# Splitting the first feed-forward network's weights on GpSimd: half a chunk in each attention step of the first batch

## What is computed

```
attn_out = sm_attn(means of 4 rows of q, k, v), each row repeated 4 times
         + local attention over |i - j| < 4                # 4 batches x 8 heads x 576 x 64
x = attn_out as 2304 x 512
h = x @ w_in;  g = max(h, 0) + alpha * min(h, 0);  x = g @ w_out      # 512 -> 2048 -> 512
h = x @ w2_in; g = where(h > 0, h, exp(min(h, 0)) - 1); out = g @ w2_out
```

## Time and profile before

| | us |
|---|---|
| median of 3 runs | 921.67 |
| lowest and highest | 920.73, 924.37 |
| the profiled execution | 921.41 |
| its span | 919.6 |
| PE busy in the span | 906.8 |
| DVE, ACT, POOL busy | 541.3, 339.1, 281.3 |

### The profile page before, as it was taken

One profiled execution on the slowest core, in us unless ns is written; L12 is line 12 of the kernel. 1 busy time (PEld: TensorE's weight loads), 2 busy tenths in 40 slices (PEclk: granted clock), 3 DMA queues, 4 the chain that ended last, 5 costly groups with the idle time before them and its releaser, 6 DMA issues.

```text
span 919.6 us, 15263 instructions
## 1 busy us (share of the span) xinstructions
PE 906.8 (99%) x5611; PEld 850.2 (92%) x5616; DVE 541.3 (59%) x1071; ACT 339.1 (37%) x784; POOL 281.3 (31%) x399
## 2 busy tenths in 40 slices
PE   8799999999999999999999999999999999999998
PEld 6689999999999999999999998888888888988887
DVE  6665656555655554454455575656865657756563
ACT  6763335334534232241232142323442324423233
POOL 3799882111210145546466541110011100000000
PEclk9999999999999999999999999999999999999999
DMA  7665442222210123544453243444464443634411
GB/s 167 144 159 146 123 123 54 54 54 54 51 44 15 29 64 124 179 131 129 157 198 90 62 145 115 115 117 117 121 183 116 115 121 111 190 117 115 115 47 69
DMA packets 119834, 100.70 MB, mean 109 GB/s; under 512 B 66000, under 2 KB 82384, under 8 KB 119760
## 3 DMA queue, kind: packets, MB, share of 16 engines
q1 hardware_dynamic: 118576, 99.42, 38.3%
q10 hardware_dynamic: 1184, 0.30, 0.2%
HBM read 80.29 MB, written 19.40 MB: 108 GB/s over the span
## 4 chain that ended last, share of the span: by engine, by line
PE 94%; POOL 2%; issue 1%; DVE 1%; DMA 1%; ACT 0%; ACTq 0%; POOLq 0%; DVEq 0%
PE ps L242 29%; PE ps L244 28%; PE ps L243 28%; PE ps L441 3%; PE ps L485 1%; PE ps L423 1%; PE ps L431 1%; PE ps L472 1%; PE ps L456 1%; PE ps L448 1%; DMA qk_nat<-in_k 1%; POOL p_l L702 1%; PE ps L438 0%; POOL p_c L699 0%; POOL w_in_lo L732 0%
## 5 line engine op out<-in xcount | busy, mean ns | idle before, releaser
L244 PE MATMUL ps<-common,w_hi 128*128 128x384 f32 x768 | 258.2, 336 | 0.0
L243 PE MATMUL ps<-common,w_hi 128*128 128x384 f32 x768 | 257.9, 336 | 0.0
L243 PEld LDWEIGHTS ps<-common,w_hi 128*128 128x128 f32 x768 | 144.6, 188 | 0.0
L244 PEld LDWEIGHTS ps<-common,w_hi 128*128 128x128 f32 x768 | 144.3, 188 | 0.0
L242 PE MATMUL ps<-common,w_out_lo 128*128 128x384 f32 x384 | 132.9, 346 | 0.5 <-DVE common L321 0.5
L242 PE MATMUL ps<-common,w_in_lo 128*128 128x384 f32 x384 | 132.7, 345 | 0.0
L317 ACT ACTIVATE common<-act_g 128x384 fp32r<-128x384 f32 x96 | 50.4, 525 | 215.4 <-PE ps L244 125.5
L883 ACT ACTIVATE act_g<-act_g 128x384 f32<-128x384 f32 x96 | 50.5, 526 | 195.1 <-DVE act_g L879 195.1
L242 PE MATMUL ps<-w_hi,common 128*128 128x512 f32 x288 | 113.6, 394 | 0.0
L244 PE MATMUL ps<-w_hi,common 128*128 128x512 f32 x288 | 113.5, 394 | 0.0
L243 PE MATMUL ps<-w_out_lo,common 128*128 128x512 f32 x288 | 113.5, 394 | 0.0
(11 more groups left out here) (104 smaller groups left out, 1533.3 us busy)
## 6 DMA issues: line engine op xcount, KB each, us to landing
ring<-w_in_parts SPq DMA_DIRECT2D x168, 256.0 KB, 2.7
w_in_parts<-parts SPq DMA_DIRECT2D x8, 1280.0 KB, 5.7
qk_nat<-in_q SPq DMA_DIRECT2D x32, 144.0 KB, 2.8
v_nat<-in_v SPq DMA_DIRECT2D x16, 288.0 KB
out<-xT SPq DMA_DIRECT2D x18, 256.0 KB, 2.3
qk_nat<-in_k SPq DMA_DIRECT2D x30, 144.0 KB, 3.1
v_win<-in_v SPq DMA_DIRECT2D x64, 67.5 KB
xT<-in_moe_w_in SPq DMA_DIRECT2D x16, 256.0 KB, 3.2
```

What stands on the lines that cost most here:

```text
L243: pe.matmul(psum, l_hi, r_lo, start=False, stop=False)
L244: return pe.matmul(psum, l_hi, r_hi, start=False, stop=stop)
```

## The change

Hi and lo of one half of a chunk are now one function, `split_weights(gp, c, which)`, with which = 0 for `w_in` and 1 for `w_out`. `w_hi_done` is raised once per half, `w_split` still once per chunk, by the second half. In step u of the first batch POOL splits half of a chunk: chunk u // 2, half u % 2. So chunks 0 and 1 are split in the first batch. The other fourteen are split in the steps 4 to 7: LATE becomes [2 to 5], [6 to 9], [10 to 13], [14, 15]. SP loads chunk 2 in step 1 and chunk 3 in step 3, as late chunks, and in the steps 4 to 7 the chunks c + 2 for c in LATE instead of c + 1.

```diff
-            LATE = [range(BATCH_UNITS, BATCH_UNITS + 2),
-                    *(range(n, min(n + 4, FC)) for n in range(BATCH_UNITS + 2, FC, 4))]
+            EARLY = BATCH_UNITS // 2
+            LATE = [range(n, min(n + 4, FC)) for n in range(EARLY, FC, 4)]
...
-            def hi_of_weights(gp, c):
+            def split_weights(gp, c, which):
+
                 gp.wait_ge(w_loaded[c % WS], 32 * (c // WS + 1))
-                for which in range(2):
-                    last = gp.tensor_scalar(w_hi[:, which, c, :], w_stage[:, c % WS, which, :], 1.0, 0.0, ALU.mult, ALU.add)
-                last.then_inc(w_hi_done, 1)
-
-            def lo_of_weights(gp, c):
-
-                gp.wait_ge(w_hi_done, c + 1)
-                for which in range(2):
-                    for cols in (slice(0, DM // 2), slice(DM // 2, DM)):
-                        last = gp.tensor_tensor((w_out_lo if which else w_in_lo)[:, c, cols], w_stage[:, c % WS, which, cols],
-                                                w_hi[:, which, c, cols].bitcast(F32), ALU.subtract)
-                last.then_inc(w_split, 1)
+                gp.tensor_scalar(w_hi[:, which, c, :], w_stage[:, c % WS, which, :], 1.0, 0.0, ALU.mult, ALU.add)\
+                    .then_inc(w_hi_done, 1)
+                gp.wait_ge(w_hi_done, 2 * c + which + 1)
+                for cols in (slice(0, DM // 2), slice(DM // 2, DM)):
+                    last = gp.tensor_tensor((w_out_lo if which else w_in_lo)[:, c, cols], w_stage[:, c % WS, which, cols],
+                                            w_hi[:, which, c, cols].bitcast(F32), ALU.subtract)
+                if which:
+                    last.then_inc(w_split, 1)
...
                 for u in range(BATCH_UNITS):
-                    step_loads(u, (), [u + 1] if u + 1 >= WS else [])
+                    step_loads(u, (), [(u + 1) // 2 + 1] if u % 2 else [])
                 for u in range(BATCH_UNITS, UNITS):
                     late = LATE[u - BATCH_UNITS] if u < 2 * BATCH_UNITS else ()
-                    step_loads(u, [c + 1 for c in late if c + 1 < FC], ())
+                    step_loads(u, [c + WS for c in late if c + WS < FC], ())
...
                     normalise(gp, u + 1)
                     sum_v(gp, u + 1)
-                    hi_of_weights(gp, u)
-                    lo_of_weights(gp, u)
+                    split_weights(gp, u // 2, u % 2)
                 for u in range(BATCH_UNITS, UNITS):
                     for c in LATE[u - BATCH_UNITS] if u < 2 * BATCH_UNITS else ():
-                        hi_of_weights(gp, c)
-                        lo_of_weights(gp, c)
+                        for which in range(2):
+                            split_weights(gp, c, which)
```

More of the change, by code:

```diff
@@ L708, in attention_then_two_ffns @@
                 .rearrange("p (s k n) -> p s k n", s=WS, k=2)
-            LATE = [range(BATCH_UNITS, BATCH_UNITS + 2),
-                    *(range(n, min(n + 4, FC)) for n in range(BATCH_UNITS + 2, FC, 4))]
-            assert len(LATE) == BATCH_UNITS and LATE[-1].stop == FC
+            EARLY = BATCH_UNITS // 2
+            LATE = [range(n, min(n + 4, FC)) for n in range(EARLY, FC, 4)]
+            assert len(LATE) == BATCH_UNITS
             FIRST_AHEAD = 2
```

## The result

The changed kernel takes 934.16 us (median of 4 runs, 932.0 to 936.32) against 921.81 us (4 runs, 920.73 to 924.37) for the kernel before: a ratio of 1.0148 with a 95% interval of 1.0117 to 1.0179, 12.4 us more. The profiled execution is the quickest of the four, 932.0 us with a span of 930.2 us, 10.6 us over the span of before.

The account below looks back on a forecast made before the run. Dense PE work bounds the kernel, so a delay before the first ffn arrives whole at the end. 0 + 2.9 + 5.95 + 0 + 1.6 = 10.45 us on 921.41 us gave 931.9, range 927.5 to 935.5.

Parts of the forecast that it names:

- the likeliest case: Whole kernel: PE waits for the late v windows and for chunk 1 at the ffn; 931.9 us, chance 0.72.
- Step 1: First batch: half of each split leaves POOL, which was idle before each normalise, so 0 us.
- Rival B: First batch: POOL's split bounds the steps, normalise 4 comes 6.2 us sooner; 921.2, not slower; chance 0.06.
- Step 2: First batch, step 2: v windows stand behind chunk 2's load on SP; reciprocal before normalise 4 2.9 us late (0.5 to 4.3).
- Rival A: First batch: windows come in time or slack swallows their delay, only the ffn wait costs; 929.0; chance 0.12.
- Step 3: Start of ffn: chunk 1 is whole only after normalise 4, so PE waits 5.95 us.
- Step 4: After PE's wait for chunk 1: a half-clock stretch costs 1.6 us, bounds 0 and 2.2.
- Step 5: Beside the ffn: chunks 2 to 5 are split in time, normalise 5 hides with some 2 us to spare; 0 us.
- rival C: Beside the ffn: four splits before normalise 5 also wait for loads, PE stops 1.8 us; 935.3; chance 0.10.

Follow-up runs that it names:

- the second profile of the same kernel: The changed kernel run again, unaltered, beside the runs of later experiments; 933.61 us, 1.0134 of the kernel before.
- with the windows ahead: Changed kernel with SP issuing the windows of v ahead of the late chunk load in the first batch; 928.14 us, 1.0099 of the kernel before.
- with chunk 1 whole: Changed kernel with chunk 1 split whole in step 2 and nothing split in step 3; 927.99 us, 1.0092 of the kernel before.
- with both edits: Changed kernel with v windows issued ahead of the late chunk load and chunk 1 split whole in step 2; 923.50 us, 1.0043.
- with two whole chunks: Kernel before with chunks 0 and 1 split whole in steps 0 and 1, the rest as 3, 4, 4, 3 beside the ffn; 928.68 us, 1.0092.
- with all mended: Changed kernel: v windows before chunk load, chunk 1 whole in step 2, gaps filled with matmuls, later chunks as 3, 5, 4, 2; 919.27 us, 0.9981.
- the kernel with only the windows late: Kernel before with one SP wait added, holding chunk 2's load until the sum of v of step 2; 922.66 us, 1.0027.
- the experiment that filled the wait: Changed kernel with 27 matmuls on constants on PE just ahead of its wait for chunk 1; 932.03 us, 1.0141 of the kernel before.

## Why the prediction was right, by its steps

The range of 927.5 to 935.5 held 934.16, and the likeliest case was the one that happened: both waits came, where they were expected. The sum by its terms, in the profiled executions:

| term | predicted | measured | from |
|---|---|---|---|
| less splitting in the steps | 0 | -0.1 a step, contained in the next row | 9.63 against 9.72 us |
| windows late, up to normalise 4 | 2.9 | 2.0 | 58.45 against 56.49 |
| wait for chunk 1 | 5.95 | 5.9 | (65.43 - 58.45) less (57.55 - 56.49) |
| clock after it | 1.6 | 2.7 | 6.32 against 61.17 - 57.55 = 3.62 |
| chunks beside the ffn | 0 | 0 | 10.6 us at 71.75 and at the end |
| sum | 10.45 | 10.6 | |

That the sums agree to 0.15 us is luck: the windows are 0.9 us below, the clock 1.1 us above, and the second profile of the same kernel has 1.6 us for the clock. The mechanism is what held, and the wait for chunk 1.

*Step 1* held: the normalises are released by DVE, and POOL's saved time turned into idle time. Rival B is excluded by the kernels that split less in the first batch and are not faster: with the windows ahead, with chunk 1 whole, with both edits, with two whole chunks, and with all mended. The row at 39.41 agrees with the Trainium skill, SBUF — State Buffer, section Who interferes with whom, on which instructions contend: the half that no longer runs beside DVE's split of x took 1.41 us, where the pair that did took 2.14. The trace does not agree with the Trainium skill's rule there on who blocks, by which the one that issues second does. In the trace of before POOL's second subtraction of that pair was issued at 42.2, ahead of DVE's split of x at 42.54, and it took 1.45 us instead of 0.72. The split of x took 0.55 us there and also at 42.62 in the changed kernel, where POOL was idle.

*Step 2* had the right mechanism and four errors that partly cancel, 2.0 us instead of 2.9. First, the chunk was issued at 40.84, not 42.35, since the changed kernel's execution ran at full clock from 24.5 to 34.2, while the sum carried along the half-clock stretch of the trace of before: 1.5 us less. Second, the windows flew longer: 6.4 us from the chunk's issue to PE's first product with them where the sum had 5.35, outside my bound of 5.75, and 7.5 us in the kernel with only the windows late: 1.1 us more, so that these outputs began at 47.26 and not at 47.7. Third, all of the outputs ran at half clock and took 50.52 - 47.26 = 3.26 us instead of 1.96; I had added 0.3 for it, and it was 1.3. Fourth, from the transposes to the end of the reciprocal,

```profile
58.12 0.25 DVE L624 RECIPROCAL stats<-stats 96x15 f32<-96x15 f32 x1
```

it took 58.37 - 50.52 = 7.85 us, not 9.3: the clock was back at 1.00, and PE did not stop for POOL between the transposes, 1.0 us to the scores instead of 1.65.

The row that I bounded the flight with, a DMA share of 0.10, was taken in another step. The estimate by the Trainium skill, DMA: Bandwidth & Descriptors, section on the anatomy of one DMA, came nearer: its 2.2 us after the last issue made 6.1 us of it. But the Trainium skill states its fixed 2.0 us there for transfers that GpSimd issues, and these are SP's. In the five executions with this wait PE began 2.7 to 4.1 us after the end of the last issue, so none agrees with 2.2. Rival A, that this delay would be swallowed, is excluded by the kernel with only the windows late.

*Step 3* was right to 0.1 us. It could be exact because it is a plain chain on one engine, counted from the normalise; the same term, 69.13 - 62.16 - 1.06 = 5.9 with normalise 4 at 62.16, stands in the second profile of the kernel.

*Step 4* was undersized for the profile: 1.6 predicted with bounds of 0 and 2.2, and 2.7 measured, 2.6 by the experiment that filled the wait. The clock was still at 0.50 for 5.6 us after PE resumed, not for 3.2. The length of that stretch is not fixed by the wait: in the second profile the clock was back 3.3 us after PE resumed, and the cost was the predicted 1.6. The upper bound of 2.2 was too low for two of the three executions (2.7, 2.4 and 1.6).

*Step 5* was right: PE has no new wait from 75 us on. Its sum counts both sides from the moment chunk 1 is whole, and the experiment that filled the wait bears it out at full clock: 1.6 us to spare before the transposes of step 5, about 2 predicted. The four chunks took longer than the sum's 17.7 us, 84.10 - 65.28 = 18.8 in the changed kernel, with one of rival C's waits for a load, 1.34 us, in it. Even so there was room: PE came to the transposes at 88.66, 2.7 us of that by the slow clock, and 88.66 - 2.7 = 86.0 is still 0.9 us behind the earliest end of the normalise, 84.10 + 0.91 (an estimate from these rows). Without the wait for chunk 1 the room is gone: in the kernels with chunk 1 whole and with both edits PE waits 2.0 us for normalise 5. There rival C's delay is real, by the fourth chunk alone. The sixteen added instructions of this step are not in the trace: POOL has 399 in both pages, and a half only adds waits.

The profiles also leave out the spread. Of the 12.4 us between the first medians 10.6 lie between the profiles; the median of the changed kernel is 2.2 above its profiled run, and that of before 0.4 above its own. In the second set the changed kernel's median, 933.61, is 1.6 above that first profiled run, and the median of before, 919.77, is 1.6 below its own: 13.8 us. In the two slowest runs of the changed kernel's first four the mean granted clock was 0.985 and 0.987, against 0.993 and 0.992 in the quicker two. Nor is 10.6 us the price against an undisturbed execution: both profiles have two half-clock stretches in the first batch. Where none came before the windows' wait, in the kernels with chunk 1 whole and with the filled wait, normalise 4 followed normalise 3 after 15.52 and 16.05 us; in the changed kernel's profile it was 13.02, and 9.7 in a step without a wait.

## What to carry to other kernels

Before taking work off an engine that another one waits for, look at what ended that engine's own idle time just before the awaited instruction; if it was idle, the work was free where it was. When a step is cut in halves, follow the semaphore that only the last half raises: who waits for it, and above all what stands behind that waiter in its queue, here the windows of v behind a weight load on SP. And a wait on TensorE can cost more than its own length, through the slow clock after it; where it can't be removed, matmuls on constants in the gap may be cheaper than the idle time, and in this kernel they made 12 runs agree within 0.8 us. Before a sum is made from two profiles, compare their granted clocks stretch by stretch.

## What the runs showed of the hardware

- Idle gaps of PE of only 1.4 us, between pieces of work with a few gaps of 0.25 us, were in some executions followed by a half-clock stretch and in others not: spans of the kernel before were 916.8 us at a granted clock of 1.00 and 919.6 us at 0.996. With 1.07 us of each gap filled, the clock was 1.00 in 11 of 12 runs and 0.999 in one.
- After a standstill of 5.76 us PE worked at half clock for 5.6 us, after one of 5.75 us in the same kernel for 3.3 us, and after one of 5.31 us, with the windows ahead, for 5.0 us. Of two waits of 2.5 us in one execution one was followed by half clock and the other was not.
- With POOL's second subtraction issued ahead of DVE's split of x, POOL's took 1.45 us instead of 0.72, and DVE's 0.55 as without POOL.
- Windows of 0.3 MB behind a 0.5 MB chunk load took 6.4 to 7.5 us from the chunk's first issue to use, in five executions with loads of v, q and k issued right behind them in each. In the trace of before the same transfers, behind loads of q and k and with nothing issued behind them until 40.31, left the DMA engines idle from 40.5 on, 6.0 us after the chunk's issue at 34.48 (granted clock, DMA share, GB/s):

```profile
40.00:40.50 0.50, 1.00 0.25 46
40.50:41.00 0.50, 1.00 0.00 0
```

This fits loads behind that slow those ahead, but it was not tried by itself.
